# A masked Gram matrix on one core: its right-hand side made narrow by a GpSimd copy, computed in two steps in later slots, and the halves of an inverse taken one slot earlier

## The reference

```python
def _attn_ref(q, k, v, beta):                     # 4 batches x 8 heads, 768 steps, D = 48
    k_n = k / (norm(k) + 1e-6)
    for t in range(S):
        y[:, :, t] = q_t . state                  # state is D x D per head
        v_old = state . k_t
        state = state + beta_t * k_t (v_t - v_old)^T
x = _moe_ref(y rearranged to 3072 x 384)          # leaky ReLU layer, 384 -> 2048 -> 384
out = _moe2_ref(x)                                # skip gate, one of 8 experts by argmax, 384 -> 1024 -> 384
```

## Time and profile before

| | us |
|---|---|
| median of 3 runs | 887.37 (886.68 to 888.38) |
| the profiled execution, its own time | 887.79 |
| its span, first to last instruction | 886.0 |
| TensorE busy in the span | 776.4 (88%) |
| VectorE, ScalarE, GpSimd busy | 661.4, 496.1, 416.3 |
| one turn (from one `up` of tile 0 to the next) | about 48 |

### The profile page before, as it was taken

The page is one execution under the profiler, slowest core; times in us unless marked ns, Lnnn a source line. Parts: engine busy times, 40 slices in busy tenths (PEclk is TensorE's granted clock), DMA queues, the critical chain, the costliest instruction groups (busy, mean ns, idle before and its releaser), DMA issues.

```text
span 886.0 us, 27697 instructions
## 1 busy us (share of the span) xinstructions
PE 776.4 (88%) x10782; PEld 624.0 (70%) x10783; DVE 661.4 (75%) x1333; ACT 496.1 (56%) x1108; POOL 416.3 (47%) x498
## 2 busy tenths in 40 slices
PE   0134689999999999999999999999999899999985
PEld 0134567777878787777787788878777677778764
DVE  6758978888888888888888787866868773553382
ACT  4543566667676767666666666555465552442261
POOL 5212254545362636354554535352353665565473
PEclk9995799999999999999999999999999999999998
DMA  9869666676777697767677676336515864363100
GB/s 214 222 115 209 130 103 115 131 132 128 131 133 147 135 138 148 128 129 135 129 130 123 129 138 123 77 66 208 180 29 205 273 231 157 104 197 113 40 17 17
DMA packets 357245, 119.76 MB, mean 135 GB/s; under 512 B 330418, under 2 KB 348388, under 8 KB 356752
## 3 DMA queue, kind: packets, MB, share of 16 engines
q1 hardware_dynamic: 351424, 104.33, 56.6%
q0 software_dynamic: 3200, 7.64, 2.6%
q10 hardware_dynamic: 2512, 6.29, 2.1%
HBM read 63.53 MB, written 21.25 MB: 96 GB/s over the span
## 4 chain that ended last, share of the span: by engine, by line
PE 35%; DVE 23%; issue 11%; ACT 9%; DMA 9%; SPq 7%; POOL 5%; DVEq 0%; POOLq 0%; ACTq 0%
PE b_acc L848 8%; PE b_h L742 7%; PE b_acc L755 7%; PE b_h L835 6%; DVE stage L1484 4%; PE b_ch L681 4%; SPq L497 3%; DVE inv L1410 3%; DVE inv L1416 3%; DMA t_dram<-inv 3%; ACT ga L953 2%; ACT operands L953 2%; DMA operands<-t_dram 2%; ACT stage L1073 1%; PE b_gr L643 1%
## 5 line engine op out<-in xcount | busy, mean ns | idle before, releaser
L1908 POOL TENSOR_TENSOR stage<-stage 128x256 f16<-128x256 f32 x192 | 143.1, 746 | 251.2 <-ACT stage L953 250.3
L742 PE MATMUL b_h<-stage,wt 128*128 128x256 f16 x1728 | 222.3, 275 | 7.9 <-DVE stage L1343 5.4
L755 PE MATMUL b_acc<-wt,stage 128*128 128x384 f16 x1152 | 219.3, 327 | 2.5 <-POOL stage L1908 1.6
L742 PEld LDWEIGHTS b_h<-stage,wt 128*128 128x128 f16 x1728 | 159.1, 98 | 28.7 <-DVE stage L1343 7.5
L755 PEld LDWEIGHTS b_acc<-wt,stage 128*128 128x128 f16 x1152 | 107.0, 98 | 57.6 <-POOL stage L1908 4.5
L953 ACT ACTIVATE stage<-stage 128x256 f16<-128x256 f32 x192 | 80.0, 417 | 106.5 <-DVE stage L1484 105.5
L1484 DVE SCALAR_TENSOR_TENSOR stage<-b_h,stage 128x256 f32<-128x256 f32 x192 | 80.7, 420 | 42.1 <-ACT stage L1073 40.6
L848 PE MATMUL b_acc<-wt,operands 128*128 128x384 f16 x552 | 98.8, 330 | 7.3 <-DVE operands L1524 7.3
L835 PEld LDWEIGHTS b_h<-y,wt 128*128 128x128 f16 x1656 | 93.5, 98 | 6.5 <-issue 4.6
L835 PE MATMUL b_h<-y,wt 128*128 128x128 f16 x1656 | 96.5, 220 | 1.5 <-DVE y L1343 0.7
L1416 DVE TENSOR_REDUCE inv<-inv 128x30 f32<-128x90 f32 (+4 forms) x180 | 85.0, 472 | 5.8
(11 more groups left out here) (215 smaller groups left out, 1289.0 us busy)
## 6 DMA issues: line engine op xcount, KB each, us to landing
operands<-in_moe_w_dram SPq DMA_DIRECT2D x18, 1536.0 KB, 7.3
a_sys<-a_dram SPq DMA_DIRECT2D x24, 256.0 KB, 4.4
kc<-operands SPq DMA_DIRECT2D x22, 256.0 KB, 4.3
natq<-in_q_dram SPq DMA_DIRECT2D x24, 192.0 KB, 4.0
raw_v<-in_v_dram SPq DMA_DIRECT2D x24, 192.0 KB, 4.1
stage<-y SPq DMA_DIRECT2D x96, 48.0 KB, 2.0
x_dram<-stage SPq DMA_DIRECT2D x24, 192.0 KB, 2.9
out_dram<-stage SPq DMA_DIRECT2D x24, 192.0 KB, 3.4
```

The lines of the kernel that those rows point to most:

```text
L742: mm = pe.matmul(b_h[f % 2][:, 0:GT], wt[0][:, a, d * FF + f * P:d * FF + (f + 1) * P], xT[:, g % 2, b, d, :], start=(i == 0), stop=(i == ...
L755: mm = pe.matmul(b_acc[w][:, 0:DM], g16[:, f % 4, a, w * P:(w + 1) * P], wt[1][:, b, f * DM:(f + 1) * DM], start=(f == 0 and (a, b) == PAR ...
L1908: pool.tensor_tensor(g16[:, f % 4, LO, :], g32[:, f % 4, :], g16[:, f % 4, HI, :], ALU.subtract).then_inc(g_lo, 1)
```

## The change

1. GpSimd copies the 64 columns that count of each of q's transposes into `kc` (`compact_q`, two copies of 64 partitions x 2048 fp16 elements, one in slot 10 and one in slot 11, behind `hidden_low`). `kc` is thus used by k and by q in turn; `compact_k` waits for `gram_p`.
2. `gram_p` takes `kc` as right-hand side: 64 columns a matmul, eight units a step, two steps in slots 13 and 14, ahead of `down`. Nothing between the two heads is computed any more, and the mask is a plain triangle.
3. VectorE masks twice instead of four times (slots 13 and 14). ScalarE's high halves are four copies on 64 partitions (slots 14 and 15), GpSimd's low halves four subtractions on 64 partitions (two in slot 15, one each in slots 0 and 1 of the next turn).
4. From turn 1 on, `inverse_high` and `inverse_low` stand in slot 11 instead of 12. On ScalarE that is ahead of `rows_out`. SyncE issues `inverse_out` ahead of `blocks_back`. ScalarE's `seed` stands in slot 13 instead of 14.
5. Index constants of the router, which lie in `kc`, are made a turn later.

```diff
@@ PE
+            def gram(bank, rhs, g, u0, u1):
+                for u in range(u0, u1):
                     for a, b in PARTS:
+                        mm = pe.matmul(bank[:, (u - u0) * C:(u - u0 + 1) * C], kT[g % 2][:, a, u, :], rhs[:, b, u, :],
+                                       start=(u == u0 and (a, b) == PARTS[0]), stop=True, skip_group_check=True)
-            def gram_p(g, st):
-                pe.wait_ge(q_turned, 32 * g + 32)
-                if st >= 2:
-                    pe.wait_ge(pm_ready, B * g + st - 1)
...
-                gram(qT, g, st).then_inc(gp_done, 1)
+            def gram_p(g, s):
+                pe.wait_ge(qc_copied, 2 * g + 2)
...
+                gram(b_gram[s], qTc, g, s * 2 * PAIRS, (s + 1) * 2 * PAIRS).then_inc(gp_done, 1)
@@ PE, turn
-                    if nxt and f == 12:
-                        gram_p(g + 1, 2 if g else 1)
+                    if nxt and f in (13, 14):
+                        gram_p(g + 1, f - 13)
                     if down_at(g, f):
...
-                    if nxt and f in ((10, 11, 13) if g else (11, 13, 14)):
-                        gram_p(g + 1, f - (10 if g else 11))
@@ ACT, turn
-                    if nxt and f == 12:
-                        inverse_high(g + 1)
-                    if nxt and 12 <= f < (15 if g else 16):
-                        p_high(g + 1, f - (11 if g else 12))
+                    if g == 0 and f == 12:
+                        inverse_high(1)
+                    if nxt and f >= 14:
+                        p_high(g + 1, f - 14, 0)
                     if up_at(g, f):
                         hidden(*up_at(g, f))
-                    if nxt and f == 11 and g:
-                        p_high(g + 1, 0)
+                    if nxt and f >= 14:
+                        p_high(g + 1, f - 14, 1)
+                    if nxt and g and f == 11:
+                        inverse_high(g + 1)
...
-                    if ahead and f == 14:
+                    if ahead and f == 13:
                         seed(g + 2)
@@ DVE, turn
-                    if nxt and (11 if g else 12) <= f < (15 if g else 16):
-                        gram_p(g + 1, f - (11 if g else 12))
...
+                    if nxt and f in (13, 14):
+                        gram_p(g + 1, f - 13)
...
                     if inv and end > mid:
                         inverse(n, mid, end)
+                    if nxt and g and f == 11:
+                        inverse_low(g + 1)
@@ POOL
+            def compact_q(g, x, before):
+                if x == 0:
+                    pool.wait_ge(q_turned, 32 * g + 32)
+                    pool.wait_ge(ga_done, min(B * (g + 2), B * G))
+                if before:
+                    pool.wait_ge(g_lo, FT * before[0] + before[1] + 1)
+                h = slice(C * x, C * x + C)
+                pool.tensor_copy(qTc[h], qT[h, :, :, h]).then_inc(qc_copied, 1)
+                pool.wait_ge(qc_copied, 2 * g + x + 1)
@@ POOL, turn
-                    if nxt and (11 if g else 12) <= f < (15 if g else 16):
-                        p_low(g + 1, f - (11 if g else 12))
+                    if nxt and f == 15:
+                        p_low(g + 1, 0, 0, up_at(g, f - 1))
                     if up_at(g, f):
                         hidden_low(*up_at(g, f))
+                    if nxt and f == 15:
+                        p_low(g + 1, 0, 1, up_at(g, f))
+                    if nxt and f in (10, 11):
+                        compact_q(g + 1, f - 10, up_at(g, f))
+                    if scan and g and f < 2:
+                        p_low(g, 1, f, up_at(g, f))
@@ POOL, before the turns
+            pool.wait_ge(nat_ready, 3)
+            for x in range(2):
+                compact_q(0, x, None)
```

More of the change, by code:

```diff
@@ L231, in build @@
         kc_copied = sem("kc_copied")
+        qc_copied = sem("qc_copied")
         kc_loaded = sem("kc_loaded")
@@ L446, in compact_k @@
                 sp.wait_ge(ga_done, B * g)
+                if g >= 2:
+                    sp.wait_ge(gp_done, 2 * (g - 1))
                 for x in range(2):
@@ L578, in turn @@
                     load_k(g + 4)
-                if is_group(g + 2):
+                if g == 0:
+                    blocks_back(2)
+                if is_group(g + 1):
+                    inverse_out(g + 1)
+                if is_group(g + 2) and g:
                     blocks_back(g + 2)
                 if is_group(g + 1):
-                    inverse_out(g + 1)
                     inverse_back(g + 1)
@@ L637, in _ @@
         def _(pe):
-            def gram(rhs, g, st):
-                n = rhs.shape[3]
-                for p in range(PAIRS):
-                    u = st * PAIRS + p
+            def gram(bank, rhs, g, u0, u1):
+                for u in range(u0, u1):
                     for a, b in PARTS:
-                        mm = pe.matmul(b_gram[st % 2][:, p * n:(p + 1) * n], kT[g % 2][:, a, u, :], rhs[:, b, u, :],
-                                       start=(p == 0 and (a, b) == PARTS[0]), stop=True, skip_group_check=True)
+                        mm = pe.matmul(bank[:, (u - u0) * C:(u - u0 + 1) * C], kT[g % 2][:, a, u, :], rhs[:, b, u, :],
+                                       start=(u == u0 and (a, b) == PARTS[0]), stop=True, skip_group_check=True)
                 return mm
@@ L986, in kn_high, with p_high @@
                 copy(kn[g % 3][h, HI, :, C * x:C * x + D], natk[h]).then_inc(kn_hi, 1)
-            def p_high(g, st):
-                act.wait_ge(pm_ready, B * g + st + 1)
-                if g:
-                    act.wait_ge(y_done, 2 * g)
-                copy(units(pT, HI, st), pm[st % 2][:]).then_inc(p_hi, 1)
+            def p_high(g, s, x):
+                if x == 0:
+                    act.wait_ge(pm_ready, 2 * g + s + 1)
+                    if g:
+                        act.wait_ge(y_done, 2 * g)
+                    else:
+                        act.wait_ge(const_pool, 3)
+                h, u = slice(C * x, C * x + C), slice(s * 2 * PAIRS, (s + 1) * 2 * PAIRS)
+                copy(pT[h, HI, u, C * x:C * x + C], pm[s][h].rearrange("p (u c) -> p u c", c=C)).then_inc(p_hi, 1)
             def a21_high(g):
@@ L1249, in _ @@
                 gram_out(1, st)
-            for st in range(2):
-                p_high(0, st)
+            for x in range(2):
+                p_high(0, 0, x)
             for x in range(2):
                 kn_high(2, x)
-            for st in range(2, B):
-                p_high(0, st)
+            for x in range(2):
+                p_high(0, 1, x)
             seed(1)
@@ L1557, in turn @@
                         inverse(n, at, mid)
-                    if nxt and f == 12:
-                        inverse_low(g + 1)
+                    if g == 0 and f == 12:
+                        inverse_low(1)
                     if gate and f in (13, 14):
@@ L1751, in _ @@
             dve.wait_ge(beta_ready, 1)
-            for st in range(B):
-                gram_p(0, st)
+            for s in range(2):
+                gram_p(0, s)
             split_w_out(0)
@@ L1893, in kn_low, with p_low @@
                 pool.wait_ge(kn_ready, 2 * g + x + 1)
-            def p_low(g, st):
-                pool.wait_ge(p_hi, B * g + st + 1)
-                u = slice(st * PAIRS, (st + 1) * PAIRS)
-                pool.tensor_tensor(pT[:, LO, u, :].rearrange("p u i -> p (u i)"), pm[st % 2][:],
-                                   pT[:, HI, u, :].rearrange("p u i -> p (u i)"), ALU.subtract).then_inc(p_ready, 1)
+            def compact_q(g, x, before):
+                if x == 0:
+                    pool.wait_ge(q_turned, 32 * g + 32)
[5 more added lines that the diff above has]
+                pool.wait_ge(qc_copied, 2 * g + x + 1)
+            def p_low(g, s, x, before):
+                pool.wait_ge(p_hi, B * g + 2 * s + x + 1)
+                if before:
+                    pool.wait_ge(g_lo, FT * before[0] + before[1] + 1)
+                h, u, c = slice(C * x, C * x + C), slice(s * 2 * PAIRS, (s + 1) * 2 * PAIRS), slice(C * x, C * x + C)
+                pool.tensor_tensor(pT[h, LO, u, c], pm[s][h].rearrange("p (u c) -> p u c", c=C), pT[h, HI, u, c],
+                                   ALU.subtract).then_inc(p_ready, 1)
+                pool.wait_ge(p_ready, B * g + 2 * s + x + 1)
             def s_low(g, r):
@@ L1988, in _ @@
             tri(before16[:], 0, -1, 1, P, ALU.is_gt, 0.0)
-            m = mask_p[:].rearrange("p (u c) -> p u c", c=P)
-            link(pool.affine_select(out=m, in_=m, pattern=[[0, PAIRS], [1, P]], compare_op=ALU.is_gt, fill=0.0,
-                                    base=0, channel_multiplier=-1))
-            m = mask_p[0:C, :].rearrange("p (u c) -> p u c", c=P)[:, :, C:P]
-            link(pool.memset(m, 0.0))
+            for h in range(2):
+                m = mask_p[C * h:C * h + C].rearrange("p (u c) -> p u c", c=C)
```

(12 more changed lines are left out.)

42 lines of the change are left out of this document (23 added, 19 removed).

## The result

| | before | changed |
|---|---|---|
| median (lowest to highest), same chip | 887.32 (886.68 to 888.38) | 938.24 (936.69 to 939.6) |
| ratio, 95% interval | | 1.0563 [1.0536, 1.059] |
| the profiled execution's own time | 887.8 | 937.11 |
| its span | 886.0 | 935.4 |

A forecast was written before the change was run, and what follows sets the result against it. TensorE was taken to set the pace. Waits of 3.65 + 1.3 + 1.0 less savings of 1.3 and 0.85 gave 3.8 us a turn, 38 in all, -1 at the start: 925 us from 887.8, range 898 to 953.

The forecast's parts named there:

- What TensorE saves.: Gram matmuls of 64 columns save 1.3 us a turn; with vanished waits, 2.15 us together.
- "recovered" 0.85: TensorE's waits for the reloaded inverse and q's transposes vanish, giving back 0.85 us a turn.
- rows_out behind the inverse: Slots 11 to 12: TensorE's first down waits 3.65 us a turn, as rows_out follows the inverse's copy-delayed high half.
- The Gram step behind the second copy: Slot 13: TensorE waits 1.3 us a turn before the first Gram step for GpSimd's second copy.
- The scan: Slots 15, 0 and 1: moved p_low meets VectorE's differences, costing 1.0 us a turn, between nothing and 3.0.
- The start: Before turn 0: mask waits go, two copies precede k's halves; between -3 and +2 us, taken as -1.
- (3): Sign: the 60-element product in slot 11 lasts 1.5 to 1.9 us, where its twin takes 0.28.
- (5): Sign: TensorE waits 3 to 4 us before the first down and 1 to 1.5 us before the first Gram step.
- (6): Sign: a turn lasts 51 to 52 us instead of 47.9.
- The saving stands: Rival: moved work fits the other engines' slack and TensorE's saving is gained, 865 us; chance 0.08.
- Cheap and dear copies: Rivals: GpSimd copies of 1.04 us, 898 us, chance 0.16; or 4.1 us, 970 us, within a case of chance 0.13.
- full loss in the scan: Rival: 3.0 us a turn lost in the scan, no waits recovered, 953 us; chance 0.13 shared with 4.1 us copies.

The follow-up runs named there:

- e10: e9 with the halves of the inverse back in slot 12: 883.71 us, 0.9952 of the kernel before.
- e8: e6 with Gram steps, masks, high and low halves one slot earlier, Gram steps in slots 12 and 13: 889.99 us, 1.0017 of the kernel before.
- e9: e8 with GpSimd's four low halves of p one slot earlier, in slots 13 and 14: 884.34 us, 0.9962 of the kernel before.
- e1: Changed kernel with the inverse's high half behind rows_out and hidden_high in slot 11 on ScalarE: 919.2 us, 1.0352 of the kernel before.
- e2: Changed kernel with both halves of the inverse back in slot 12: 919.53 us, 1.0374 of the kernel before.
- e7: Kernel before with only the inverse's halves moved to slot 11, ahead of rows_out on ScalarE: 895.69 us, 1.0089 of the kernel before.
- e4: Changed kernel with each GpSimd copy cut to 8 of 16 units from group 1 on: 917.75 us, 1.0343 of the kernel before.
- e5: Changed kernel with q's copies made by two SyncE DMAs instead of GpSimd from group 1 on: 916.61 us, 1.0331 of the kernel before.
- e11: Changed kernel with 18 unread matmuls filling TensorE's wait before the first down in turns 1 to 9: 935.41 us, 1.0496 of the kernel before.
- e3: Changed kernel without GpSimd's four low halves of p from group 1 on: 922.07 us, 1.0385 of the kernel before.
- e6: e5 with the inverse's high half behind hidden_high of tile 1 in slot 11: 890.98 us, 1.0036 of the kernel before.
- e12: e1 with 12 unread matmuls ahead of the Gram step of slot 13 in turns 1 to 9: 916.04 us, 1.0279 of the kernel before.

## Why the prediction was right, and where it was short

- **What TensorE saves.** 48 Gram matmuls of 64 columns take 2 x 0.70 = 1.4 us a turn, as said; 1.3 is saved. The "recovered" 0.85 is too high. Seven turns of the changed kernel (`gate_s` at 170.84 to `gate_s` at 541.01) take 370.17, 52.9 each against 47.9: 5.0 more. The costs found are 3.49 + 1.50 + 1.71 = 6.7, so the savings were 1.7 and not 2.15. One reason is the rows: the earlier trace rows are waits of the weight loads, and a part of those passes while matmuls still run. TensorE's matmuls themselves waited less in the same 350 us of the kernel before (130 to 480 us):

```profile
PE b_ch L681 <- DMA operands<-t_dram: 3.0, 6, 0.8
PE b_gr L643 <- DMA operands<-nq: 0.7, 2, 0.6
```

In the seven turns that match (164.48 to 499.86 before) it is 5.0 us, 0.7 a turn. The other is a wait that grew: L1353 held `up` for 2.6 us in these turns before and for 4.8 now, 0.3 a turn more. Together 1.3 + 0.7 - 0.3 = 1.7. And the reason given for the 0.85, the inverse stored earlier, is not borne out (e10; with it stored early, e8 and e9 still wait 2.3 and 2.5 us for it in 490); the waits may have gone because the turns got longer, which wasn't separated.
- **rows_out behind the inverse: 3.65 forecast, 3.49 measured.** Reckoned as the forecast did, from the end of an `up` of 0.98, it is 321.24 - 316.60 - 0.98 = 3.66; the bracket counts from the end of the last matmul's record. e1, e2 and e7 show that the order makes it, e4 and e5 that the copy's hold on the product is 1.17 of it. The copy took 1.89 for 1.85 forecast, the product 1.37: the one-input rate of GpSimd from two other sizes of the earlier trace rows was good to 2%. The forecast let the product run for 0.28 after the copy; it ended 0.07 after it, as the earlier trace rows had shown (301.64 behind 301.57).
- **The Gram step behind the second copy: 1.3 forecast, hardly a trace of it in the changed kernel.** The copy ended at 324.55, as reckoned to 0.2, but TensorE, slowed by 1.29 us, came only at 324.81. In its place stand 1.5 for the clock, which the forecast did not have. e11 shows the wait at full clock, 1.00, and e1 one of 2.19 where the first wait doesn't precede it. So the queue was understood, but that this term of the sum was near what was lost here is luck: another loss of about its size lay over it.
- **The scan: 1.0 forecast, 1.71 measured**, 1.48 of it `p_low`'s (e3). The step that was mis-sized. "I take 1.0, a third: the copies' wait has let the other engines catch up by then" was a guess between far ends, and its reason doesn't hold: in e1, with another wait ahead, and in e6, with neither wait, z is waited for as long, 1.2 us. VectorE's two-input differences run beside the low halves of p wherever these stand in slots 0 and 1. The second difference of z took 1.03 in the changed kernel (at 338.18, above), and before:

```profile
315.94 0.53 DVE L1436 TENSOR_TENSOR z<-scan,z 128x384 f16<-128x384 f32 x1
```

- **The start: -1 forecast, about +1.4 measured.** The 5.47 of the earlier trace rows did go, but 4.34 for the copies and 4.11 for u came instead, and a copy held the Gram step of turn 0 for 2.14. `gate_s` of turn 1 starts 6.4 us later than before, of which 5.0 are put down to the first slow turn.
- **The sum.** Turns 1 to 8 lose 5.0 each for the forecast's 3.8. Turns 9 and 10, with the shorter waits, lose 8.9 together. Ten turns make 48.7 for 38, the start 1.4 for -1, and 0.7 comes back behind them: 887.8 + 48.7 + 1.4 - 0.7 = 937.2, where the profiled execution took 937.1. Of the 1.2 a turn, 0.7 is the scan, 0.4 the savings, 0.2 the clock in place of the second wait, less 0.15 at `rows_out`.
- **What was to be seen:** (1), (2), (4) and (7) as written; (3) with 1.37 instead of 1.5 to 1.9; (5) half, the second wait hidden; (6) 52.7 to 53.2 instead of 51 to 52.
- **The rivals.** "The saving stands" failed at `leaky` of tile 1, as argued: the product starts behind it. Cheap and dear copies are out by the 1.89. Of the "full loss in the scan", 3.0, a little over half came.

## What to carry to other kernels

Taking 1.3 us from the engine that sets the pace is gained only if what it waits for next is ready; here the moved work put two queues in front of it. Before an operation is moved ahead of another on an in-order engine, ask what that other feeds: `rows_out` feeds TensorE at once, the inverse's halves only a turn later, and swapping the two was worth 19 us (e1). And a low half that is needed in slot 1 must be asked for where its high half is ready, not where a slot is free: that one slot was e8's 1.0017 against e9's 0.9962 of the kernel before.

## What the hardware showed that was not expected

- **The clock falls behind a wait.** After 3.49 us without work TensorE was granted 0.50, the lower of its two levels, for the next 2.2 us and 0.81 in the 1.8 after that, or fell a microsecond later; after shorter waits it fell in some turns only: five of eight after 2.32 us (e5), two of eight after 2.64 (e4), four of eight after 2.19 (e1; 0.57 over 4 us where it fell). After e7's 1.38 it was 1.00 (130 to 620 us). With the waits filled it didn't fall there (e11 and e12: 1.00 from 130 to 570 us). The price was 1.5 us a turn in the changed kernel, and 1.1 from one turn of e1 to the other.
- **Two losses in one place don't add.** The lower clock and the wait for the copy lay over each other: taking the first away gave 0.4 us a turn (e11), since the second took its place.
- **The two-byte copy on GpSimd runs at the rate of the four-byte ones:** 1.887 us for 2048 elements a partition, (1.887 - 0.190) / 2047 = 0.83 ns an element, against 0.81 in the earlier trace rows. VectorE makes it in 1.04.
